# Second slot and last output products of a retention and gated MLP kernel, put in another order

## The reference

```python
# retention: B=2, H=8 heads, S=768, D=64
for t in range(S):
    state = gamma * state + einsum('bhd,bhe->bhde', k[:, :, t], v[:, :, t])
    y[:, :, t] = D**-0.5 * einsum('bhd,bhde->bhe', q[:, :, t], state)
# token mixing of rank 32 (U 768x32, V 32x768) and a channel MLP, d_model 512, 2048 hidden
u = x + (x^T @ U @ V)^T
x = u + relu(u @ w_ch1) @ w_ch2
# spatial gating: w_in 512x1024, w_spatial 768x768, w_out 512x512
h = relu(x @ w_in);  u, v = halves of h
v_n = (v - mean(v)) / sqrt(var(v) + 1e-6)
out = (u * (w_spatial @ v_n + b)) @ w_out
```

## Time and profile before

| | |
|---|---|
| median of 3 runs | 467.58 us |
| profiled execution, its own time | 468.86 us |
| its span (first to last instruction) | 466.9 us |
| TensorE busy | 458.2 us, 98% |
| VectorE, ACT, POOL busy | 351.3, 253.6, 48.1 us |
| TensorE's clock granted, 40 slices | full in each |
| chain that ended last | TensorE 94% |
| TensorE busy, by stage | 8.25 of the first 10 us, 8.49 of the next, 9.82 of the third, then 10.00 |

### The profile page before, as it was taken

How to read it: one execution, slowest core, us unless ns; L and a number is a source line. 1 busy time by engine, 2 the same in 40 slices (tenths; PEclk the granted TensorE clock), 3 DMA queues, 4 the chain that set the end, 5 groups by cost and what they waited for, 6 DMA issues and landing times.

```text
span 466.9 us, 8670 instructions
## 1 busy us (share of the span) xinstructions
PE 458.2 (98%) x3128; PEld 409.0 (88%) x3128; DVE 351.3 (75%) x772; ACT 253.6 (54%) x592; POOL 48.1 (10%) x52
## 2 busy tenths in 40 slices
PE   8899999999999999999999999999999999999995
PEld 4788898899999999888888999988888789999995
DVE  4788879977889978874855976765813998895783
ACT  1666756546667655843464655733523765564451
POOL 2178970000000000000100000000100001000000
PEclk9999999999999999999999999999999999999999
DMA  8989801433332343201220343302105002041003
GB/s 275 406 298 333 298 3 46 136 135 136 135 126 92 127 137 97 94 24 66 91 91 1 102 130 115 108 1 91 45 1 202 1 0 93 0 155 71 0 1 136
DMA packets 20889, 51.36 MB, mean 110 GB/s; under 512 B 1520, under 2 KB 3952, under 8 KB 19568
## 3 DMA queue, kind: packets, MB, share of 16 engines
q1 hardware_dynamic: 20432, 50.29, 31.3%
q10 hardware_dynamic: 416, 0.53, 0.4%
HBM read 47.66 MB, written 3.15 MB: 109 GB/s over the span
## 4 chain that ended last, share of the span: by engine, by line
PE 94%; DVE 2%; DMA 2%; ACT 1%; issue 0%; DVEq 0%
PE bank L1615 10%; PE bank L1613 10%; PE bank L1616 9%; PE bank L1594 9%; PE bank L1596 9%; PE bank L1597 8%; PE bank L1719 3%; PE bank L1721 3%; PE bank L1722 3%; PE bank L1460 3%; PE bank L1654 2%; PE bank L1653 2%; PE bank L1655 2%; PE bank L1505 2%; PE bank L1499 2%; PE bank L1737 2%
## 5 line engine op out<-in xcount | busy, mean ns | idle before, releaser
L1594 PE MATMUL bank<-bh,w1c 128*128 128x256 f32 x336 | 94.7, 282 | 0.3 <-DVE hl L1099 0.3
L1597 PE MATMUL bank<-bh,w1c 128*128 128x256 f32 x336 | 94.7, 282 | 0.0
L1596 PE MATMUL bank<-bl,w1c 128*128 128x256 f32 x336 | 94.6, 282 | 0.0
L1615 PE MATMUL bank<-hl,w2h 128*128 128x512 f32 x192 | 75.9, 395 | 0.0
L1613 PE MATMUL bank<-hh,w2h 128*128 128x512 f32 x192 | 75.8, 395 | 0.0
L1616 PE MATMUL bank<-hh,w2l 128*128 128x512 f32 x192 | 74.7, 389 | 0.0
L1594 PEld LDWEIGHTS bank<-bh,w1c 128*128 128x128 f32 x336 | 63.5, 189 | 7.0 <-issue 0.5
L1091 DVE TENSOR_TENSOR c<-bank,p 128x256 f32<-128x256 f32 x72 | 30.4, 423 | 51.1 <-PE bank L1597 29.8
L1596 PEld LDWEIGHTS bank<-bl,w1c 128*128 128x128 f32 x336 | 63.4, 189 | 5.4
L1597 PEld LDWEIGHTS bank<-bh,w1c 128*128 128x128 f32 x336 | 63.4, 189 | 0.0
L672 ACT ACTIVATE p<-bank 128x256 f32<-128x256 f32 x72 | 27.5, 381 | 45.4 <-PE bank L1597 44.3
(11 more groups left out here) (179 smaller groups left out, 948.3 us busy)
## 6 DMA issues: line engine op xcount, KB each, us to landing
w1raw<-w SPq DMA_DIRECT2D x24, 512.0 KB, 5.3
w2raw<-w SPq DMA_DIRECT2D x24, 512.0 KB, 4.1
att<-attn SPq DMA_DIRECT2D x7, 1152.0 KB, 7.8
att<-attn SPq DMA_DIRECT2D x10, 384.0 KB, 5.7
out_T<-stage SPq DMA_DIRECT2D x7, 384.0 KB, 2.5
wsp_raw<-w_sp SPq DMA_DIRECT2D x1, 2304.0 KB, 9.1
winraw<-w_in SPq DMA_DIRECT2D x4, 512.0 KB, 4.9
tab<-decay SPq DMA_DIRECT2D x7, 258.0 KB, 5.0
```

The source lines that it names most:

```text
L1594: mm(o, w1c[k][:, 0, q, s], bh[:, q, c, :], start=(opens and c == 0), stop=False, skip_group_check=True)
L1596: mm(o, w1c[k][:, 0, q, s], bl[:, q, c, :], start=False, stop=False, skip_group_check=True)
L1597: m = mm(o, w1c[k][:, 1, q, s], bh[:, q, c, :], start=False, stop=(c == 1), skip_group_check=True)
L1615: mm(ch_ps[c][:, :], w2h[h][:, s], hl[k][:, h, :], start=False, stop=False, skip_group_check=True)
```

## The change

- In slot i = 1 ACT makes both xT copies of pair 0 and the first score copy ahead of the key decays of pair 1, and rounds U behind the second score copy.
- In slot i = 1 VectorE masks the first scores before decay_q(1), makes the four first states before the xn rests, then the last state and the second mask, and U's rest behind that.
- In slot i = 1 TensorE runs down(0) between the two output halves instead of ahead of both.
- POOL's mask waits for the table of decays.
- Output products 4 and 5 change places, with their roundings, rests, copies and sums; the sums of w_out are rounded in the order 0, 1, 3, 2. The third sum is counted and stored in two halves, and each half of the last product waits for the half of the sum that frees its bank.

```diff
@@ outside the engines
-        ORDER = (0, 3, 2, 1, 4, 5, 6)
-        ORDER_B = (0, 3, 2, 1, 4, 5, 6)
+        ORDER = (0, 3, 2, 1, 5, 4, 6)
+        S_ORDER = (0, 1, 3, 2)
@@ sync
-            for n, (i, j) in enumerate(((0, 0), (1, 1), (0, 1))):
-                sp.wait_ge(oc_sum, n + 1)
-                store_block(i, j)
-            for m in range(2):
-                sp.wait_ge(last_sb, m + 1)
-                sp.dma_start(out[2 + m, :, S:S + HS], stage[:, 2 + m, 0:HS]).then_inc(stored, 16)
+            for j in range(2):
+                sp.wait_ge(oc_sum, j + 1)
+                store_block(0, j)
+            for j in (1, 0):
+                for m in range(2):
+                    if j:
+                        sp.wait_ge(oc_sum, 3 + m)
+                    else:
+                        sp.wait_ge(last_sb, m + 1)
+                    sp.dma_start(out[2 + m, :, S + j * HS:S + (j + 1) * HS], stage[:, 2 + m, j * HS:(j + 1) * HS]
+                                 ).then_inc(stored, 16)
@@ gpsimd
             def mask_b(i):
+                pool.wait_ge(tab_loaded[i % 2], 16 * (i // 2) + 16)
@@ scalar
             xt_copy(0, 0)
-            decay_k(1)
             xt_copy(0, 1)
-            act.wait_ge(cst_loaded, 16)
-            nc.scalar.activation(ust[:, :, :], urep[:, :, :], ACT.Copy).then_inc(ust_hi, 1)
             for i in range(1, NI):
                 sc_copy(i, 0)
+                if i == 1:
+                    decay_k(i)
                 xn_copy(i - 1, 0)
                 xn_copy(i - 1, 1)
                 sc_copy(i, 1)
+                if i == 1:
+                    act.wait_ge(cst_loaded, 16)
+                    nc.scalar.activation(ust[:, :, :], urep[:, :, :], ACT.Copy).then_inc(ust_hi, 1)
...
-                act.wait_ge(op_done, 7 + m)
+                act.wait_ge(op_done, 8 + m)
...
             copy_op(0)
-            round_os(2)
-            round_ob(4)
+            round_os(3)
             round_ob(5)
             copy_op(1)
+            round_ob(4)
+            round_os(2)
             copy_op(2)
-            round_os(3)
             round_ob(6)
@@ vector
             mask_a(0, 1)
-            decay_q(1)
             for i in range(1, NI):
                 mask_a(i, 0)
+                if i == 1:
+                    decay_q(i)
+                    states(i, 0, NC - 2)
+                xn_rest(i - 1, 0)
+                xn_rest(i - 1, 1)
+                if i > 1:
+                    states(i, 0, NC - 2)
+                states(i, NC - 2, NC - 1)
+                mask_a(i, 1)
                 if i == 1:
                     (U's rest, unchanged)
-                xn_rest(i - 1, 0)
-                xn_rest(i - 1, 1)
-                if i == 1:
-                    mask_a(i, 1)
-                states(i, 0, NC - 2)
-                states(i, NC - 2, NC - 1)
-                if i > 1:
-                    mask_a(i, 1)
                 p_rest(i - 1)
...
             def sum_oc(n):
-                ps, p, i, j = ((zo_ps, po1, 0, 0), (xo_ps, po5, 1, 1), (yo_ps, po16, 0, 1))[n]
+                ps, p, i, j = ((zo_ps, po1, 0, 0), (yo_ps, po16, 0, 1), (xo_ps, po5, 1, 1))[n]
                 dve.wait_ge(op_done, 4 + n)
-                dve.wait_ge(op_copied, (1, 2, 3)[n])
+                dve.wait_ge(op_copied, (1, 3, 2)[n])
...
                 for m in range(2):
+                    if n == 2 and m:
+                        dve.wait_ge(op_done, 7)
                     k = nc.vector.tensor_tensor(stage[:, 2 * i + m, j * HS:(j + 1) * HS], ps[m][:, 0:HS], p[:, m, :],
                                                 ALU.add)
-                k.then_inc(oc_sum, 1)
+                    if n == 2 or m:
+                        k.then_inc(oc_sum, 1)
...
             rest_ob(1)
+            rest_os(3)
+            rest_ob(5)
+            rest_ob(4)
             rest_os(2)
-            rest_ob(4)
-            rest_ob(5)
-            rest_os(3)
             sum_oc(0)
@@ tensor
-                down(i - 1)
+                if i > 1:
+                    down(i - 1)
                 outputs(i, 0)
+                if i == 1:
+                    down(i - 1)
                 outputs(i, 1)
                 up(i - 1)
...
-                if q == 6:
-                    pe.wait_ge(oc_sum, 2)
                 for m in range(2):
+                    if q == 6:
+                        pe.wait_ge(oc_sum, 3 + m)
...
-                    if m == 1 or q == 6:
+                    if m == 1 or q == 6 or q == 4:
                         i.then_inc(op_done, 1)
```

More of the change, by code:

```diff
@@ L494, in store_block @@
                              stage[:, 2 * i:2 * i + 2, j * HS:(j + 1) * HS]).then_inc(stored, 16)
-            for n, (i, j) in enumerate(((0, 0), (1, 1), (0, 1))):
-                sp.wait_ge(oc_sum, n + 1)
-                store_block(i, j)
-            for m in range(2):
-                sp.wait_ge(last_sb, m + 1)
-                sp.dma_start(out[2 + m, :, S:S + HS], stage[:, 2 + m, 0:HS]).then_inc(stored, 16)
+            for j in range(2):
[9 more added lines that the diff above has]
+                                 ).then_inc(stored, 16)
             for c in range(CT):
                 sp.wait_ge(stage_free[c], 16)
-            sp.wait_ge(stored, 16 * (CT + 1))
+            sp.wait_ge(stored, 16 * 6)
         @block.gpsimd
@@ L1328, in rest_os @@
             def rest_os(s):
-                dve.wait_ge(os_hi, s + 1)
+                dve.wait_ge(os_hi, S_ORDER.index(s) + 1)
                 nc.vector.tensor_tensor(os_block(wout2_rest, s), os_block(wout2, s), raw(osh)[:, s, :, :],
@@ L1347, in rest_ob @@
             def rest_ob(q):
-                dve.wait_ge(ob_hi, ORDER_B.index(q) + 1)
+                dve.wait_ge(ob_hi, ORDER.index(q) + 1)
                 if q in T_OF:
@@ L1745, in out_product @@
                 if q in S_OF:
-                    pe.wait_ge(os_lo, S_OF[q] + 1)
+                    pe.wait_ge(os_lo, S_ORDER.index(S_OF[q]) + 1)
                     wh, wl = osh[:, S_OF[q], :, :], os_block(wout2_rest, S_OF[q])
@@ L1750, in out_product @@
                     wh, wl = w_out_block(wouth, i, j), w_out_block(woutl, i, j)
-                pe.wait_ge(ob_lo, ORDER_B.index(q) + 1)
+                pe.wait_ge(ob_lo, ORDER.index(q) + 1)
                 if q in T_OF:
```

## The result

The changed kernel takes 469.54 us (median of 5, 469.11 to 470.51) against 467.58 (467.53 to 468.03): ratio 1.0048, interval 1.0034 to 1.0061. It is slower by 1.96 us, clear of the 0.2% that can be told.

What follows compares the result with a forecast made beforehand. TensorE, busy 98% of the span, was taken as the bound. Slot i = 1 at +1.81 us and the tail at 0, added to 467.58, gave 469.4 us, with 467.8 to 470.2 for 8 in 10.

Steps and rivals of the forecast that it cites:

- Until kv: Slot i = 1 up to kv: ACT's new order moves kv from 16.93 to 15.67, a gain of 1.26 us.
- Outputs, down, up: Slot i = 1 after kv: down waits for U's rest, up moves from 21.38 to 23.19.
- rival B: Slot i = 1: VectorE or loads are quicker, down hardly waits; +0.3 us or less, 467.8 us; chance 0.06.
- The step to +1.81: Slot i = 1 as a whole: up starts at 23.19 instead of 21.38, costing 1.81 us, bounds 1.3 to 2.6.
- Two terms, U and V: Slot i = 1: TensorE idles 1.5 us for U's rest before down and 0.9 for V's rest before up.
- Later slots as a block: Slots behind i = 1: no new waits, all move together by +1.81 us.
- Tail at 0: Output products and stores at the end: no change in time, bounds +0.2 and -1.7 us.
- the tight wait of the last product: Last product's second half waits for the last sum: fits by 0.15 us, else costs up to 0.2.
- two guesses for a last store free of the fetch: Final 192 KB store without the instruction fetch ahead: lands in about 2.0 us, or 2.45 by the skill's fit.
- Rival A: End of kernel: last store comes free of the instruction fetch, 1.2 to 1.7 us off, 467.9 us; chance 0.19.
- Rival C: V or the next table lands late, or TensorE's clock falls in the 1.5 us pause: +3 us, 470.6; chance 0.07.
- the case's 468.9 to 470.2: Whole kernel: span of times for the prediction's main case, slower, given 0.64.

Runs made afterwards that it cites:

- the pair with one slot: Two kernels with one faster slot i = 1 (U's and V's rests on POOL, three states behind xn rests), new tail against old: 467.24 and 466.82 us.
- best_new_tail: Changed kernel with V rounded ahead of p, U's and V's rests on POOL, three states behind the xn rests in slot i = 1: 467.24 us, ratio 1.0001.
- down_first: Changed kernel with down again ahead of both output halves on TensorE, ACT's and VectorE's orders as changed: 471.32 us, ratio 1.0085.
- act_only: Kernel before with ACT's order alone changed (U rounded right behind key decays) and POOL's new wait, VectorE and TensorE as before: 467.63 us, ratio 1.0015.
- down_first_busy: Changed kernel with down ahead of both output halves, plus 24 idle matmuls of zeros ahead of down: 475.96 us, ratio 1.0186.

## Why the prediction was right

469.4 us was forecast, 469.54 measured, slower as forecast. By its steps, all counted from the first scores:

- **Until kv**: a gain of 1.26 was worked out, kv at 2.56; measured 2.54. Masks, score copy and key decays came as laid out. decay_q cost TensorE nothing.
- **Outputs, down, up**: 4.1, 6.93 and 10.08 were worked out; measured 4.05, 6.78 and 9.97. The order of VectorE's row gave the number: each instruction took its old duration in its new place. (Against rival B the prediction counts six VectorE instructions between kv and U's rest; by its own steps, and in the trace, they are eight.) The step to +1.81 was 0.11 high against the same trace, and 0.12 low against a run whose table lands early.
- **Two terms, U and V**, each shown by taking it away: 0.85 and 0.84 us.
- **Later slots as a block**: shown, no new wait turned up behind slot 1; last copy 1.81 later.
- **Tail at 0**: TensorE's work is unchanged there, and the tight wait of the last product held. But the term was sized wrongly: the pair with one slot gives +0.4 for the new tail, outside its stated bound of +0.2. I had looked at TensorE's place in its stream and said that the fetch would come at the same time; in best_new_tail it moved before 461.2, ahead of the last copy at 461.39, not behind it, and in the changed kernel's profile none moved until the last store had landed. Slot and tail as the experiments give them add up to 2.1 to 2.3 us, and 1.96 was measured, with an interval of 1.6 to 2.9. That the forecast came within 0.15 us is in part luck, since it left out a tail of 0.4; that nearly all of the loss is the slot's is not luck. The prediction's two guesses for a last store free of the fetch were about 2.0 and an estimate of 2.45 us; 1.9 to 2.0 were measured.
- **Rival A** (the fetch spares the last store) did happen in the changed kernel's profile, and the span shows it, but the median of the timed runs does not. The likely reason is that the timed runs of before mostly had no such fetch in the way either: on the later chips its spans were 464.2 to 466.5, mostly about 465, not 466.9. They have no profiles, so this is inferred. The row was right; its use as the normal case, by these spans, was wrong.
- **Rival B** was out: down waited 1.4 us. **Rival C**: the clock held through 1.4 us, and down_first shows that the danger was real and near.

The chances were added up a hundredth off: A and B make 0.25 for no change, not 0.24, and with all of the case's 468.9 to 470.2 above the 0.2% (468.5) nothing is taken off the 0.71. It changes nothing.

The gain that the ACT order makes is real at kv and void at up, because up waits for VectorE's row, which the ACT order does not shorten; act_only showed it alone.

## What to carry to other kernels

Follow a constant's preparation to its consumer on every engine it passes: U and V are needed once, were rounded with idle ACT time, and cost 0.85 us each only since U's rest stood last in a full VectorE row and V's behind p. Where TensorE must wait, several short pauses with work between can be cheaper than one long one: here 0.7, 1.4 and 0.8 us left the clock full, and 3.4 in one piece cost another 1.6. Compare profiles between fixed points inside the kernel, and don't read a span's last two microseconds as the kernel's.

## What the runs showed of the hardware

- The clock fell after a pause of 3.4 us (down_first), and TensorE then worked for 3.4 us at half before it rose: 1.6 us lost. Pauses of up to 1.4 us did nothing. The Trainium skill (TensorE: Matmul & The Clock Gate, Part 1) describes two states of this clock gate, 1.2 and 2.4 GHz, set by how busy TensorE has been recently; the traces agree, 0.50 and 1.00.
- A plain f32 matmul of 128x256 took 0.43 us in down_first_busy, and appears twice in the count (48 for 24); one of the six fp32r matmuls of down, of the same shape, took 0.16.
- POOL's mask of 128x384, 1.0 us elsewhere, took 1.58 beside decay_q, which kept its 0.82; in the changed kernel:

```profile
14.46 1.58 POOL L527 TENSOR_TENSOR am<-am,tab 128x384 f32<-128x384 f32 x1 [3.49 <-ACT am L612]
16.43 1.00 POOL L527 TENSOR_TENSOR am<-am,tab 128x384 f32<-128x384 f32 x1 [0.39 <-ACT am L612]
```
